# Sixteen unread 512-column products on TensorE between the source sums and the first transposes

## The reference

```python
def _moe_ref(x, w_gate, w_output_gate, w1, w2):
    logits = x @ w_gate
    e_idx = np.argmax(logits, axis=1)
    ...
    for e in range(E):
        mask = e_idx == e
        h = np.maximum(x[mask] @ w1[e], 0.0)
        ye = h @ w2[e]
        out[mask] = gate_w[mask, None] * eom[mask, e, None] * ye

def _moe2_ref(x, w_in, w_out):
    h = x @ w_in
    g = np.maximum(h, 0.0) + np.log1p(np.exp(-np.abs(h)))
    return g @ w_out
```

## Time and profile before

| what | us |
|---|---|
| median of 3 runs | 797.38 |
| lowest and highest of them | 792.86, 800.24 |
| the profiled execution's own time | 794.79 |
| its span | 793.1 |
| TensorE busy in it | 742.5 |
| VectorE busy in it | 408.9 |
| mean granted TensorE clock | 0.972 |

### The profile page before, as it was taken

One profiled execution on the slowest core, in us unless ns is written; L12 is line 12 of the kernel. 1 busy time (PEld: TensorE's weight loads), 2 busy tenths in 40 slices (PEclk: granted clock), 3 DMA queues, 4 the chain that ended last, 5 costly groups with the idle time before them and its releaser, 6 DMA issues.

```text
span 793.1 us, 14615 instructions
## 1 busy us (share of the span) xinstructions
PE 742.5 (94%) x5156; PEld 681.5 (86%) x5157; DVE 408.9 (52%) x858; ACT 378.0 (48%) x950; POOL 231.6 (29%) x230
## 2 busy tenths in 40 slices
PE   7999945999999999996799999999999999999996
PEld 5788734999999999996698999899999989999995
DVE  4777877456565777675543343343343334334332
ACT  6877731355454666554443443453353344335332
POOL 5333306537565578768300100010010001001001
PEclk9999975999999999999799999999999999999999
DMA  9969335545556676754000000010010001001001
GB/s 258 239 165 265 144 122 136 190 151 187 179 162 188 185 222 230 212 174 130 27 1 1 15 25 0 0 40 0 0 40 0 0 0 40 0 0 40 0 0 40
DMA packets 30082, 75.51 MB, mean 95 GB/s; under 512 B 4368, under 2 KB 12576, under 8 KB 30048
## 3 DMA queue, kind: packets, MB, share of 16 engines
q1 hardware_dynamic: 23440, 54.30, 23.1%
q0 software_dynamic: 5744, 16.04, 6.9%
q10 hardware_dynamic: 864, 4.74, 1.5%
HBM read 65.61 MB, written 9.46 MB: 95 GB/s over the span
## 4 chain that ended last, share of the span: by engine, by line
PE 90%; DVE 5%; issue 2%; ACT 1%; DMA 1%; POOL 1%; another core or an unknown queue 0%; DVEq 0%; SPq 0%; ACTq 0%; POOLq 0%
PE bank L622 13%; PE bank L624 13%; PE bank L623 13%; PE bank L646 9%; PE bank L648 8%; PE bank L644 8%; PE bank L635 4%; PE bank L637 4%; PE bank L636 4%; PE bank L521 3%; PE bank L547 3%; PE bank L532 2%; PE bank L564 2%; PE bank L608 1%; DVE w_lo L1100 1%
## 5 line engine op out<-in xcount | busy, mean ns | idle before, releaser
L1231 DVE SCALAR_TENSOR_TENSOR g_sb<-bank,soft 128x384 f32<-128x384 f32 x96 | 53.5, 558 | 242.0 <-ACT soft L917 242.0
L913 ACT ACTIVATE soft<-bank 128x384 f32<-128x384 f32 x96 | 47.2, 492 | 215.6 <-PE bank L624 214.8
L487 POOL DMA_INDIRECT out<-y_sb,out_rows_i x18 | 17.3, 962 | 387.5 <-ACT y_sb L924 383.9
L1100 DVE TENSOR_TENSOR w_lo<-raw,w_hi 128x1024 fp32r<-128x1024 f32 x68 | 93.6, 1378 | 52.2 <-ACT w_hi L835 46.0
L622 PE MATMUL bank<-x_parts,w_hi 128*128 (+1 forms) x352 | 111.6, 317 | 3.9 <-DVE w_lo L1100 3.4
L623 PE MATMUL bank<-x_parts,w_hi 128*128 (+1 forms) x352 | 110.8, 315 | 0.0
L624 PE MATMUL bank<-x_parts,w_lo 128*128 (+1 forms) x352 | 110.7, 315 | 0.0
L835 ACT ACTIVATE w_hi<-raw 128x1024 fp32r<-128x1024 f32 x68 | 71.7, 1057 | 52.5 <-PE bank L637 46.7
L635 PE MATMUL bank<-h_hi,w_hi 128*128 128x384 f32 (+3 forms) x256 | 80.6, 315 | 1.6 <-DVE h_lo L1120 1.6
L422 POOL TENSOR_SCALAR xs_sb<-landing 128x256 f32<-128x256 f32 x48 | 62.4, 1308 | 63.1 <-PE bank L608 63.1
L636 PE MATMUL bank<-h_hi,w_lo 128*128 128x384 f32 (+3 forms) x256 | 77.5, 303 | 0.0
(11 more groups left out here) (186 smaller groups left out, 1689.7 us busy)
## 6 DMA issues: line engine op xcount, KB each, us to landing
raw<-we SPq DMA_DIRECT2D x64, 512.0 KB
x_tokens<-x_sb ACTq DMA_DIRECT2D x6, 771.0 KB, 3.9
v_sb<-vw SPq DMA_DIRECT2D x12, 384.0 KB, 8.2
raw_m<-wm POOLq DMA_DIRECT2D x8, 512.0 KB, 5.3
raw<-wm SPq DMA_DIRECT2D x8, 512.0 KB
q_sb<-qT SPq DMA_DIRECT2D x12, 256.0 KB, 5.7
k_sb<-kT SPq DMA_DIRECT2D x12, 256.0 KB, 7.0
v_sb<-vw SPq DMA_DIRECT2D x4, 576.0 KB, 13.9
```

The costliest lines, as they stand in the source:

```text
L1100: nc.vector.tensor_tensor(w_lo[:, r, :], raw[:, r, :], w_hi[:, r, :].bitcast(F32), ALU.subtract).then_inc(w_lo_done, 1)
```

## The change

TensorE gets a loop of four turns with four products each, behind `block_sums` and in the same entry turn. Each product takes 128 columns of the one-hot table as weights and streams 512 columns of it, into bank 0. Nothing reads the result; the first transposes write over it later. No wait and no signal is added, and no other engine's program is touched.

```diff
+            def keep_busy():
+                onehots = place_onehot[:, :, :].rearrange("p a b -> p (a b)")
+                with pe.Fori(0, 4):
+                    for n in range(4):
+                        nc.tensor.matmul(first_t_ps[0][:, :], onehots[:, 0:P], onehots[:, 0:SLOT + P], start=True, stop=True)
+
@@
                         with pe.If_eq(kind, ENTRY):
                             block_sums()
+                            keep_busy()
```

## The result

| | before | after |
|---|---|---|
| median (20 runs each, one chip) | 796.58 | 792.32 |
| lowest, highest | 790.53, 802.57 | 784.43, 798.79 |
| ratio, 95% interval | | 0.9934 [0.9906, 0.9961] |
| profiled execution, its span | 794.79, 793.1 | 786.58, 784.8 |

The forecast was no change, 797.4 us in a range of 792.5 to 801.5, and the median came 0.2 us under that range. The ratio leaves out runs over 1.5% above the fastest of the same kernel, which are seven of the changed kernel's 20 (796.7 us and more) and one of the kernel before's; over all 20 of each the means are 792.72 and 796.08 us, a ratio of 0.9958. So the changed kernel was faster by 0.4 to 0.7%, on this chip, and its own runs spread over 14 us.

What follows compares the result with a forecast made beforehand. VectorE's own chain was taken to gate p2(0) at 140.89. Terms summed 0 + 0 + 0 = 0 on 794.79 us profiled; the median of three runs, 2.6 us above, gave 797.4 us, range 792.5 to 801.5.

Steps and rivals of the forecast that it cites:

- The products' cost at their place: Before the transposes: all 16 take at most 6.8 us at the lower clock, covered by 6.92 us idle; cost 0.
- The gate: In front of p2(0), 140.89: VectorE's own chain up to `h_lo`, no step of it waiting for a product on TensorE.
- The clock is gone again when the first products start: By 132.5, more likely than not, the high level is lost and first products run as before; gain 0.
- The first rival: Clock holds to 132.5, then falls in a 4.0 us wait before p2(0); 2.1 us slower, 799.5 to 799.7; chance 0.22.
- The second rival: Added products run into the transposes, ending later than 128.95; 0.5 to 3.1 us slower, 797.9 to 800.5; chance 0.08.
- The expert slots: Slots after 172: the prediction counts as wrong if they take longer at full clock.
- something else in the layout of TensorE's program: Remaining case, no place or size given; chance 0.03.
- the upper end for the loop: Added loop's four turns on TensorE's sequencer, each 0.95 us: +3.1 us, products ending at 132.3; value taken 0.

Runs made afterwards that it cites:

- held: The changed kernel plus 36 more unread 128-column products around the third block's transposes, VectorE's order as before; 1.0045 of the kernel before, 792.17 us on chip 5.
- One column: The changed kernel with each added product streaming 1 column in place of 512, against the kernel before on chip 10; 1.0002, 786.66 us.
- the 12.6 us on chip 11: Kernel before with VectorE's 16 routing steps moved into the first slot and GpSimd's 18 scatters spread over the slots; 0.9827, 785.97 us against 798.55.
- early scatter: Kernel before with GpSimd's 18 scatters issued two behind each half slot from slot 2; 1.0014 (chip 10), 1.0024 (chip 6), 0.9970 (chip 14).
- one column again: The changed kernel with 1 column per added product in place of 512, against the kernel before on chip 14; 0.9966, 786.91 us.
- deferred: Kernel before with VectorE's 16 routing steps moved behind the first slot's second `h_lo`, no added products; 0.9963 of the kernel before, 786.92 us on chip 5.

## Why the prediction was wrong

**What held.**
- *The products' cost at their place.* 5.71 us, ended at 128.54, 1.38 us ahead of the transposes; the clock rose on the way, at 127.1. Nothing at the loop's entry or its turns can be seen: the first product starts behind the sums without idle time.
- *The gate.* p2(0) was released by `h_lo` again, 20.88 us behind the source sums instead of 20.56, with 2.50 us of idle time in front. VectorE's chain from the third scaling on took 10.3 to 10.6 us in all 14 profiles with its order as before and no filling products; moving its steps brought p2(0) 1.5 to 3.6 us sooner than the 20.56.
- *The clock is gone again when the first products start.* It was 1.00 from 127.1 to 133.9 and 0.50 from 133.9 to 137.3. So the forecast's case came about, but its working was wrong in part: the level lived through all the transposes, and fell only at the wait behind them.
- *The first rival's price.* `held` made its wait, 3.98 us, and the expert stage lost 1.6 us of the 2.1. In the changed kernel itself the rival did not come about.
- *The second rival* did not occur in this trace: 1.38 us lay between products and transposes.
- *The expert slots*, 228.1 us both times.

**What failed** is a term that was put at nothing: everything outside the change's place. "No case moves the time by even 0.5%; what can move the measured figure more is the scatter of the kernel". That spread was taken as noise without a place. Some of it has one, the passage from the experts to the dense network: in the two profiles of the first comparison, that passage and the dense network behind it were 7.9 + 2.1 us shorter with the change, with signals of TensorE 0.70 us late instead of 5.66. The 0.03 for "something else in the layout of TensorE's program" named a faster case without a place or a price.

The change was compared five times. It gave nothing on three chips (0.9997, 1.0001, 0.9999, 12 runs each) and 0.4 to 0.7% in the two comparisons where the kernel before takes 797 to 799 us. The number of the first comparison's chip is not on record, so these two may be one chip.

Some of the miss is luck. The base of the forecast, 797.38, is the median of three runs, and 20 runs gave 796.58; the same range laid around that would have held 792.32. Two small slips changed nothing. By its own terms the upper end for the loop is 3.7 - 0.39 = 3.3 us and not 3.1, and 800.2 moved up by 1.5 is 801.7.

The open term could have been read from the trace before. The earlier trace rows hold a wait of 4.70 us at 384.6, and the prediction used it for the price of a lost clock without asking what TensorE waited for. One line of ScalarE, 386.13 with 8.23 us of idle time and the releaser a product that had ended at 380.45, says that neither engine's work was the cause. That would not have given the sign, but a size. As an estimate from that trace, 4.5 us lay between the last expert product and ScalarE's copy, 4.7 us in the wait, and 2.1 us in the clock lost by it (the prediction's price). That is 11.3 us, and a range down to 786.1 would have held the result.

**What stays open.** Why the changed kernel was faster in two comparisons and not in three. That its 20 first runs happened to hold more executions with punctual signals is not excluded, since one profile of each kernel was taken there and the changed kernel's is from its fast end. If it is the change, how 16 unread products 230 us earlier make signals less late was not found. One column against the change would have told the work from the instructions, but it was not run on chip 11, and on chips 10 and 14 there was no effect of the change to divide.

That GpSimd's scatters hold the signals up rests on four things: where both stand in time, that the held-up steps are let go as the scatters land, that no signal in the passage is late in the five profiles with the scatters moved, and the 12.6 us on chip 11. Three of the five are from chips where no profile shows a late signal at all; on chip 14 it is one profile without against three with, on chip 11 one against one. The early scatter by itself was not run on chip 11, where the loss is largest. Why some chips show nothing with the same scatters in the same place is not known.

## What to carry to other kernels

Unread products that warm up TensorE give nothing where another engine releases the next product that counts, and where they make the real products finish sooner they can cost the clock a second time, as in `held`; move the releasing engine's chain first. When a trace shows an engine waiting for a product that ended microseconds before, look for what else is being issued at that time, and try it in another place. And a difference of 0.5% found on one chip is a result about that chip until it has been seen on another.

## What the runs showed of the hardware that was not expected

- A semaphore step of TensorE can reach the trace, and the engine that waits for it, up to 6.03 us behind the end of its product (one column again), in a stretch where GpSimd issues 18 indirect DMAs in a row. On chips 10 and 6 no profile of eight has it; on 5, 14 and 11 all eight with the scatters in the old place have it, by 3.08 to 6.03 us. That the DMAs are the cause is not shown beyond the above.
- One kernel's median differs by 12.4 us (1.6%) between chips 6 and 11.
- The granted clock rose to 1.00 at 134.3 in `deferred`, when TensorE had done nothing but transposes since the source sums ended at 123.9. The Trainium skill (TensorE: Matmul & The Clock Gate, Part 4: PE-mode transpose) says that the high level does not engage for transposes. The kernel before agreed with that (0.50 through all twelve); this trace does not. In the nine other traces without unread products it rose 16.0 to 19.2 us behind the source sums' start, among the first products, and in `deferred` 11.8.
- Once at 1.00, the clock stayed there through all twelve transposes of the kernel after (127.1 to 133.9).
- Filling products behind transposes delay the transposes' signals: by 1.0 to 1.6 us in `held`, with 20 products of 128 columns behind them.
- The 16 new products of half precision start 0.427 us apart at the lower clock, as those of four-byte operands do, and 0.216 apart at the higher, where those take 0.231.
